# GpSimd's splits of the token-mixing weights at other places of its program

## What is computed

```python
# 1. attention: 8 heads of 64, a window of 128 keys and 4 sink keys
a = softmax(where(keep, scale * q @ k.T, -1e9));  x = a @ v
# 2. four attention experts; each position takes its best two
logits = x @ w_gate;  topk = argpartition(-logits, 2)[..., :2]
w = softmax over the two selected logits
for e in range(4):
    a = softmax(causal(scale * (x @ wq[e]) @ (x @ wk[e]).T))
    out += (weight of e, or 0) * (a @ (x @ wv[e]) @ wo[e])
# 3. gated dense layer with token mixing
u, v = split(gelu_tanh(x @ w_in))
v_n = (v - mean(v)) / sqrt(var(v) + 1e-6) * g_ln
v_s = einsum('ts,bsd->btd', w_sg, v_n) + b_sg[None, :, None]
return x + (u * v_s) @ w_out
```

## Time and profile before

| | us |
|---|---|
| median of 3 runs | 371.44 (371.26 to 371.63) |
| profiled execution, whole time | 371.92 |
| its span, first to last instruction | 370.1 |
| PE busy | 361.7 (98%) |
| VectorE busy | 213.0 (58%) |
| ScalarE busy | 194.7 (53%) |
| GpSimd busy | 142.8 (39%) |

### The profile page before, as it was taken

The page is one execution under the profiler, slowest core; times in us unless marked ns, Lnnn a source line. Parts: engine busy times, 40 slices in busy tenths (PEclk is TensorE's granted clock), DMA queues, the critical chain, the costliest instruction groups (busy, mean ns, idle before and its releaser), DMA issues.

```text
span 370.1 us, 7823 instructions
## 1 busy us (share of the span) xinstructions
PE 361.7 (98%) x2850; PEld 334.7 (90%) x2850; DVE 213.0 (58%) x611; ACT 194.7 (53%) x520; POOL 142.8 (39%) x188
## 2 busy tenths in 40 slices
PE   7899999999999999999989999999999999999997
PEld 5688888889999999999979898899999988999997
DVE  4887776611798763089897608524744255335342
ACT  5999999933688764478979253432310033411010
POOL 5899888896726117000725628310000032100000
PEclk9999999999999999999999999999999999999999
DMA  7865555322320000000222301000011200000112
GB/s 240 227 203 189 190 187 195 103 89 94 112 61 3 2 2 1 2 0 2 61 83 59 99 3 57 2 1 2 0 44 43 85 2 0 2 0 0 45 42 86
DMA packets 13029, 24.20 MB, mean 65 GB/s; under 512 B 1344, under 2 KB 6848, under 8 KB 12992
## 3 DMA queue, kind: packets, MB, share of 16 engines
q1 hardware_dynamic: 12992, 23.70, 20.6%
HBM read 20.55 MB, written 3.15 MB: 64 GB/s over the span
## 4 chain that ended last, share of the span: by engine, by line
PE 92%; DVE 3%; DMA 2%; issue 1%; ACT 1%; SPq 1%; DVEq 0%; ACTq 0%
PE banks L1028 15%; PE banks L1030 15%; PE banks L1029 15%; PE banks L1299 14%; PE banks L1113 6%; PE banks L1070 6%; PE banks L1082 5%; PE banks L1198 5%; PE banks L1210 5%; PE banks L1234 5%; PE banks L1124 2%; DMA qd<-in_qT 2%; PE banks L1214 1%; DVE eqL L860 1%; DVE Pa L742 1%
## 5 line engine op out<-in xcount | busy, mean ns | idle before, releaser
L566 ACT ACTIVATE Pa<-Pa,NMa 128x260 f32<-128x260 f32 (+1 forms) x96 | 46.1, 482 | 8.9 <-DVE NMa L742 8.9
L471 POOL TENSOR_TENSOR Pa<-Pa,RIa 128x520 f32<-128x520 f32 (+1 forms) x48 | 42.6, 908 | 5.9 <-DVE RIa L767 5.9
L742 DVE CUSTOM_DVE_ANT_0 Pa<-banks,win 128x260 f32<-128x260 f32 (+1 forms) x96 | 33.4, 403 | 17.3 <-PE banks L1070 16.9
L547 POOL TENSOR_TENSOR rstd<-vare,minus_half 128x1 f32<-128x1 f32 x12 | 11.9, 991 | 77.6 <-DVE vare L962 77.6
L722 ACT ACTIVATE gH<-uT 128x384 fp32r<-128x384 f32 x16 | 8.4, 526 | 49.9 <-DVE uT L981 49.9
L622 ACT ACTIVATE Pb<-Pb,NM 128x256 f32<-128x256 f32 (+5 forms) x48 | 31.7, 663 | 3.6 <-DVE NM L823 3.0
L1299 PE MATMUL banks<-w_sgL,vnH 128*128 128x384 f32 x96 | 32.5, 338 | 0.0
L979 DVE TENSOR_TENSOR vb<-banks,b_all 128x384 f32<-128x384 f32 x16 | 8.9, 558 | 37.0 <-PE banks L1299 37.0
L823 DVE CUSTOM_DVE_ANT_0 Pb<-banks,causal 128x256 f32<-128x256 f32 (+5 forms) x48 | 28.8, 620 | 1.4 <-PE banks L1198 0.2
L1070 PE MATMUL banks<-kd,qd 64*128 64x260 f32 (+1 forms) x192 | 26.2, 393 | 2.5 <-DVE NMa L742 1.3
L1210 PE MATMUL banks<-ident,Pb 128*128 128x128 f32 x168 | 24.2, 275 | 1.1 <-DVE NM L823 1.0
(11 more groups left out here) (153 smaller groups left out, 1083.6 us busy)
## 6 DMA issues: line engine op xcount, KB each, us to landing
va<-in_v SPq DMA_DIRECT2D x8, 384.0 KB, 3.6
out<-raw SPq DMA_DIRECT2D x15, 192.0 KB, 1.9
kd<-in_kT SPq DMA_DIRECT2D x7, 396.0 KB, 5.3
qd<-in_qT SPq DMA_DIRECT2D x7, 384.0 KB, 6.2
vs<-in_vsink SPq DMA_DIRECT2D x8, 336.0 KB, 4.4
raw<-in_w_sgT SPq DMA_DIRECT2D x9, 256.0 KB, 2.7
raw<-in_w_in SPq DMA_DIRECT2D x8, 256.0 KB, 2.7
raw<-in_w_b SPq DMA_DIRECT2D x8, 193.0 KB, 4.5
```

What stands on the lines that cost most here:

```text
L471: nc.gpsimd.tensor_tensor(Pa[s][:, h, ts, :], Pa[s][:, h, ts, :], RIa[:, s, h, ts].unsqueeze(2).broadcast_to((P, ts.stop - ts.start, WIN)) ...
L566: nc.scalar.activation(Pa[s][:, h, t, a:WIN], Pa[s][:, h, t, a:WIN], ACT.Exp, bias=NMa[:, s, h, t:t + 1], scale=-1.0, accum_out=RSa[:, s, ...
L742: nc.vector.tensor_tensor_reduce(out=Pa[s][:, h, t, a:WIN], in0=banks[:, score_banks(p, t)[h], 0:WIN - a], in1=m[:, :], scale=-SCALE, scal ...
```

## The change

The nine strips of w_sg are distributed differently over GpSimd's stream. Before: five strips behind the last input split, the first spread of pass 1, two strips, the second spread, two strips. Then GpSimd waited for the end of the mix (`x2_ready`), and split the four strips of w_out with one `inverse_root` behind each. After: two strips, a new wait for the gate's differences (`gate_exp_in` for both batches), two strips, the first spread, three strips, the second spread. Then, behind the wait for `x2_ready`, one `inverse_root` and one strip in turn, six times: the last two strips of w_sg and the four of w_out.

```diff
-SG_SPREAD = (5, 7)
+SG_TIMES = (2, 4, 7)
...
-            split_sg(0, SG_SPREAD[0])
+            split_sg(0, SG_TIMES[0])
+            pool.wait_ge(s_["gate_exp_in"], B)
+            split_sg(SG_TIMES[0], SG_TIMES[1])
             spread_scale(1, 0)
-            split_sg(*SG_SPREAD)
+            split_sg(SG_TIMES[1], SG_TIMES[2])
             spread_scale(1, 1)
-            split_sg(SG_SPREAD[1], SG_STEPS)
             pool.wait_ge(s_["x2_ready"], B * MIX_N)
...
-            for n in range(OUT_STEPS):
-                split_late(O_STEPS + IN_STEPS + SG_STEPS + n)
-                if n < T:
-                    inverse_root(n)
-            for n in range(min(OUT_STEPS, T), B * T):
+            for n in range(SG_TIMES[2], SG_STEPS + OUT_STEPS):
+                inverse_root(n - SG_TIMES[2])
+                split_late(O_STEPS + IN_STEPS + n)
+            for n in range(SG_STEPS + OUT_STEPS - SG_TIMES[2], B * T):
                 inverse_root(n)
```

## The result

| | before | changed |
|---|---|---|
| median, us | 371.59 (6 runs, 371.26 to 372.02) | 369.69 (6 runs, 369.26 to 369.98) |
| ratio, 95% interval | | 0.9948 (0.9936 to 0.9961) |
| profiled execution, span | 370.1 | 367.4 |
| PE busy | 361.7 | 360.2 |
| GpSimd busy | 142.8 | 143.3 |

The kernel is 0.52% faster. Of the 2.7 us between the two spans, 0.48 lie before pass 1 begins and have nothing to do with the change: the opening run of seven transposes of pass 1 stands at 176.92 in one trace and at 176.44 in the other. Traces of one and the same kernel differ there too (176.44, 176.88 and 176.50 in three traces of the changed kernel). So I measure everything from that run of seven, within one trace.

A forecast was written before the change was run, and what follows sets the result against it. PE, busy 361.7 of 370.1 us, was taken as the bound, so only closing its few idle places gains. Terms -1.71 +0.05 +0.65 -0.69 = -1.70 us, off the median 371.44, gave 369.7 us, range 368.9 to 370.7.

The forecast's parts named there:

- first stretch: Pass 1, between PE's two runs of seven transposes: w_sg splits stop holding VectorE's gate steps; gain 1.71 us.
- sg3 on L905: Pass 1, behind the gate's differences: w_sg's fourth split holds L905, VectorE 0.75 us late; cost 0.05 us.
- sg6 on the second L860: Ahead of pass 1's second spread: w_sg's seventh split holds VectorE's L860, so that spread is late; cost 0.65 us.
- end of the pass: Start of pass 1's expert mix: without w_sg's last two splits there, L860 is not held; gain 0.69 us.
- dense stage: Six splits, one behind each of GpSimd's first six square roots, may hold the last tile's L970; cost 0.
- rival (b): 0.6 us of the first stretch stays and the late collision costs 0.9 rather than 0.65: 370.5 us, chance 0.17.
- the late collision: Near 202 to 204.5 us, w_sg's seventh split and VectorE's L860 hold each other before the second spread; cost 0.65 us.
- Part two: Pass 1: w_sg's third and fourth splits placed behind the gate's differences; cost 0.05 us, bounds 0 and 0.4.
- part three: Pass 1: three w_sg splits after the first spread, none after the second; cost 0.65 us, bounds 0 and 1.5.
- rival (a): Before the second spread, GpSimd and VectorE pass each other at 202 without colliding: 369.1 us, chance 0.19.
- Rival (c): Something other than the splits holds the gate's steps in pass 1: 371.4 us, chance 0.05.
- Rival (d): Slow load of w_sg's seventh strip delays second spread and PE: 372.2 us if landing takes 5.2 us, chance 0.03.

The follow-up runs named there:

- late strips alone: Kernel before with only the last two w_sg strips moved to the dense stage, w_out's splits behind them: 371.22 us, ratio 0.9979.
- second and third series: Later timing series, each on one chip with its own runs of the kernel before; the changed kernel took 369.66 and 369.47 us.
- four strips: Changed kernel with four w_sg splits instead of three between the two spreads: 372.92 us, ratio 1.0024; again 373.14 us, ratio 1.0050.
- the memsets: Kernel before with the splits of w_sg's third to fifth strips replaced by three or five write-only memsets each: 369.96 and 370.06 us.
- the better kernel: Changed kernel with w_sg's last three strips split in the mix, behind the second spread: 369.28 and 369.20 us.

## Why the prediction was right, and where it was not

The time was forecast at 369.7 us and measured at 369.69. The terms, each against its own measurement:

| term | predicted | measured | by |
|---|---|---|---|
| first stretch | -1.71 | -1.77 | second run of seven, 13.54 to 11.77; same with the wait alone |
| sg3 on L905 | +0.05 | 0 at its place | see below |
| sg6 on the second L860 | +0.65 | +0.42 | L1214 in the changed kernel against before less 1.77; +0.44 against sg6 moved away |
| end of the pass | -0.69 | -0.80 to -0.84 | late strips alone, mix to token mixing |
| dense stage | 0 | 0 | no PE wait from 205 to 250 |
| sum | -1.70 | -2.18 to token mixing | 72.71 to 70.53 |

The mechanism was right, but for what the hold of L905 costs later on, and the agreement to 0.01 us is luck. By the traces my sum was 0.48 too small, and all four errors point the same way. The medians above differ by 1.90 us, with an uncertainty of 0.5; in the second and third series they differ by 2.25 and 2.17, as the traces do. The sum was also taken off 371.44, the median of three runs, where the six have 371.59. The second forecast, 370.2 for the profiled execution, missed: it took 369.26, of which 0.48 are the sum and 0.48 the earlier start of pass 1. Two smaller sums of the prediction are 0.1 us off and decide nothing: by its own terms rival (b) is at 370.6 and the reading with the whole L860 at 369.9.

*First stretch.* Right, and by the mechanism named: the splits hold the gate's steps and the wait removes it. ScalarE's extra copy, which the bound of 0.6 was for, costs nothing, and the late collision was cheaper than forecast and not dearer; so rival (b) is out on both counts.

*sg3 on L905.* The hold came as forecast, a little shorter (0.76 us against 0.8 to 0.9, so VectorE was 0.59 late and not 0.75), and PE did not feel it there. From the opening run to the transposes of spread 1 the changed kernel needs 19.76 us in pass 1 and 19.81 in pass 0. But the step that counted its price as 0.05 is wrong in one respect: the hold delays spread 1 by 0.6 us and sg6 by 0.5, and this is what puts sg6 on the second L860. Without the hold (the run without the wait, the only one that shows it) the late collision costs under 0.1 us. Part two had an indirect price of about 0.35 us that I had booked under part three. The argument against rival (a), that sg6 would collide even with VectorE on time, was true of the collision and wrong about the price. In that run the step L843 and the first L860 were held, and spread 2 was hardly late. Rival (a) itself, no collision at all, did not come.

*sg6.* The chain of events is as forecast: the wait for the DMA, a held subtraction, a held L860, then a late spread 2 and a gap ahead of L1214. The size was 0.42 instead of 0.65. On the clock of before (2.25 us later, the 0.48 and the 1.77) sg6 began at 201.63 against my 201.8, its subtraction ended at 204.0 against 204.1, the second L860 at 204.42 against 204.5, again 0.42 behind GpSimd, and spread 2 began at 204.59 against 204.67. Then spread 2 took 1.76 us instead of the 1.99 that I had carried over, since L928 was ahead of it by more (it started 0.25 us before the spread, 0.04 in the kernel before). In other traces the same pairs go together: 0.04 ahead with 1.98 us (sg6 behind the mix), 0.25 ahead with 1.76 (without the wait), and 1.47 us where L928 is over before the spread begins (four strips). Those two, 0.08 and 0.23, make spread 2 end 0.31 earlier than I had it; 0.08 are lost again, since PE's weight load came 0.12 us behind that end and not 0.04. This is the difference of 0.23. If the Trainium skill's rule that the later of the two fully blocks (SBUF — State Buffer, Who interferes with whom) is read as a whole L860 of 0.56 us behind GpSimd's end, the trace does not agree with it: it was 0.42.

*End of the pass.* Too small by 0.11 to 0.15. To the first matmul of the mix the gain was as forecast: from L1214 it is 3.51 us in the changed kernel and 4.21 before, 0.70 less. I had taken the time between the last matmul and the first of the mix, and not that after a wait the second matmul follows in 0.29 us instead of 0.18; the trace of before shows that, and without the wait they follow in 0.17.

*Dense stage.* Right: L970 of the last tile was held to 242.06 and the token mix began at 246.97.

Rival (c), that the change does not do what it says, is out by the wait alone and by the memsets. Rival (d) did not occur: sg6 began at 201.63 on the clock of before, as a load of 2.7 us has it. The fourth strip shows roughly its rate, 1.99 us at spread 2's start and 1.69 at PE; no run had a slow load alone.

## What to carry to other kernels

A small instruction of VectorE that falls on a long one of GpSimd can take the length of the long one: 1.07 us instead of 0.17 beside a subtraction of 1.29. So look in the profile for tiny operations whose time ends with a neighbour engine's instruction, and compare the same line in a repeat of the loop where that neighbour is idle. When work is moved off such a place, follow everything behind it on its engine: here a hold that cost nothing at its own place shifted later work by 0.6 us onto a step that PE did wait for, and the better kernel put that work where VectorE has nothing to do. Distances between fixed instructions within one trace repeated to 0.1 us, so that an effect of 0.4 us could be told, while the ratios of whole executions carry 0.5 us of uncertainty and more.

## What the runs showed that I had not expected

- A PE idle of 2.1 us at one place went with a mean granted clock of 0.994 or 0.995 in 12 of 16 executions, and with some 2 us more (in the second series 372.71 and up against 370.87 to 371.67 of the same kernel at 1.000). All the other kernels had 6 such executions in 114, the changed one with its 0.44 us of idle there none in 16. So an idle place may cost twice its length. Where the clock falls was not seen.
- GpSimd instructions that only write (memset) do not hold VectorE's two-input instructions: 0.26 and 0.25 us in the two cases that lie wholly within one memset, against 0.55 to 1.33 beside a split in the kernel before.
- About one us of delay of VectorE's gate steps (L919 at 1.10 us with the wait alone, 0.12 undisturbed) can stop short of PE at one place, while 0.8 us at another reaches PE as 0.42.
